# First linear attention of a fused attention chain: tile semaphores, another order of the products, other banks

## The chip, the cores and the metric

The kernel runs on one core of one Trainium2 chip. The metric is the device time of one execution in microseconds. The core has TensorE (PE), VectorE (DVE), ScalarE (ACT), GpSimd (POOL) and SyncE (SP), each with its own instruction queue in program order, and 16 DMA engines. The engines synchronise by semaphores.

## The reference

The computation is a chain over 8 batches of 576 positions. It has three stages; the first is the one that the change touches.

```python
kv  = einsum('bhsd,bhse->bhde', k, v)            # 8 heads of 64: one 64x64 state per head
out = einsum('bhsd,bhde->bhse', q, kv)           # linear attention
x   = out / sqrt(mean(out*out, -1) + 1e-6) * g_norm

# second stage: 4 experts, each a causal attention of head size 64 over x,
# of which the gate (x @ w_gate, two highest of four) mixes two
q, k, v = x @ wq[e], x @ wk[e], x @ wv[e]
ye = softmax(causal(q @ k.T / 8)) @ v @ wo[e]

# third stage
h = gelu(x @ w_in);  u, v = halves of h
v_s = w_sg @ layernorm(v) + b_sg                 # mixes positions
return x + (u * v_s) @ w_out
```

All inputs and the output are float32. In the third stage x stands for the output of the second.

## The kernel before, in words

The sequence of a batch is padded from 576 to 640 rows, five tiles of 128. The kernel is written with an order of work per batch ("part"), a list of units such as `("o", 3)`; every engine runs through the same list and does its own share of each unit, so the list sets the order on every queue. Part -1 is the opening (the list `FIRST`, line 79): it prepares the first batch and combines weights. Parts 0 to 7 are the batches; each ends with the first linear attention of the next batch.

PSUM is used in six slots: `w0` and `w1` of two banks each and `t0` to `t3` of one bank each. The class `Slots` (line 28) gives each unit a slot and counts two semaphores per slot: `full` is raised by PE when the unit's last matmul is done (`finish`), `free` by the engine that evicts last (`give`). PE waits in `dst` until the slot's former unit is evicted. In the opening the slots are written out in `FIRST_SLOT` (line 82); in the batches the four narrow slots go round. The first four units of batch 0 are the q/k products `("qk", (m, 0))`, in the slots t3, t0, t1, t2.

The units of the opening are:

- `woT`, `w2`: the output weights of the experts are transposed and multiplied with `w_in`, so that `wo @ w_in` is one weight. `("w2", c)` for c = 0 to 3 is one chunk of the contraction (eight matmuls of 512 columns, line 1050), accumulated in w0 and w1 over all four chunks.
- `kv`: the states of all heads for a batch, in slot t3 (line 1078). DVE copies them to `kvd`.
- `qT`, j: tile j of the queries is transposed by four PE transposes (line 1029) and evicted by ACT (line 569). The five tiles come by one DMA each (lines 381 and 384), and all raise the semaphore `q_loaded`; PE waits for all five before `("qT", 0)` (line 1026).
- `o`, j: queries times states (eight matmuls in the profile, line 1092). ACT squares it (line 593), DVE sums the squares per head (line 833), POOL raises to the power -1/2 (lines 513 and 514). ACT's square of tile j waits for DVE's sum of tile j - 1. DVE scales the tile (`scale_x`, line 731) and frees the slot; it does this one `o` unit late, behind the sum of the next tile (or at a later `x` unit), and for tile t of 2 or more it waits until `("x", t-2)` has been transposed, since there are two buffers.
- `x`, j: the scaled tile is transposed (line 1100), ACT evicts its rounded high half (line 597), DVE its low half (line 840), which frees the slot. All products of x are done in three passes over high and low halves.
- `split`, name: ACT writes the high half of a weight (line 575), DVE the low half (line 815). ACT waits for all DMAs of that weight; for the q/k weights (`wqk0` to `wqk3`) these are the eight DMAs of line 432.

A q/k product (line 1118, its matmuls at the helper's line 943) waits until the x tiles that it reads are evicted, its weight's halves are ready, and its slot is free. The values' products `v` wait for the weight `wv` in the same way.

SP issues the DMAs of the opening without waiting: `wo`, two chunks of `w_in`, k and v of batch 0, the five query tiles, two more chunks of `w_in`, g_norm, the q/k weights, the value weights. Then, once `kv` is done, follow `w_sg`, `w_out` and two small vectors, and, once `("qT", 4)` is done, sixteen DMAs of query blocks of batch 1 (line 392), which also raise `q_loaded`; DVE waits for them at `turn` in batch 0 (line 912).

Of the kernel before, what the change touches and what calls it, by code (L numbers as in the profile page):

```python
# [55 lines left out]
def moe_chain(nc, q, k, v, g_norm, w_gate, wq, wk, wv, wo, w_in, g_ln, w_sg, b_sg, w_out, out):  # L56
# [3 lines left out]
    PAD = P - S % P  # L60
    SP = S + PAD
    NT = SP // P
# [14 lines left out]


    FIRST = [("woT", 0), ("woT", 1), ("w2", 0), ("w2", 1)] + [("kv", c) for c in range(DC)]
    FIRST += [("qT", 0), ("qT", 1), ("o", 0), ("qT", 2), ("o", 1), ("qT", 3), ("qT", 4), ("o", 2), ("w2", 2), ("x", 0),  # L80
              ("split", "wqk0"), ("o", 3), ("x", 1), ("split", "wqk2"), ("w2", 3), ("o", 4), ("x", 2), ("x", 3), ("x", 4)]
    FIRST_SLOT = {("kv", 0): "t3", ("qT", 0): "t0", ("qT", 1): "t1", ("o", 0): "t2", ("qT", 2): "t0", ("o", 1): "t3",
                  ("qT", 3): "t1", ("qT", 4): "t0", ("o", 2): "t1", ("x", 0): "t0", ("o", 3): "t2", ("x", 1): "t3",
                  ("o", 4): "t1", ("x", 2): "t0", ("x", 3): "t2", ("x", 4): "t3"}


    LATE_QK = {0: [("split", "wqk1")], EP: [("split", "wqk3"), ("w2e", 0)], 1: [("split", "wv")]}
# [69 lines left out]
    def units(part):  # L157
# [3 lines left out]
        def ring(unit, among):  # L161
            if part < 0:
                got.append((unit, FIRST_SLOT[unit]))
                return
# [35 lines left out]
    with ExitStack() as ctx:  # L200
# [3 lines left out]
        def sem(name):  # L204
            return ctx.enter_context(nc.semaphore(name))
# [91 lines left out]
        wv_lo = sem("wv_lo")  # L297
        wo_lo = sem("wo_lo")
        wout_lo = sem("wout_lo")
        q_loaded = sem("q_loaded")  # L300
        q_turned = sem("q_turned")
        kv_loaded = sem("kv_loaded")
# [69 lines left out]
        def _(sp):  # L372
# [6 lines left out]

            def load_q(b):  # L380
                sp.dma_start(qin[PAD:P, 0, :].rearrange("p (h d) -> p h d", h=H),
                             q[b, :, 0:PAD, :].rearrange("h s d -> s h d")).then_inc(q_loaded, 16)
                for t in range(1, NT):
                    sp.dma_start(qin[:, t, :].rearrange("p (h d) -> p h d", h=H),
                                 q[b, :, P * t - PAD:P * (t + 1) - PAD, :].rearrange("h s d -> s h d")
                                 ).then_inc(q_loaded, 16)

            def load_q_blocks(b):

# [279 lines left out]
        def _(dve):  # L669
# [4 lines left out]
            def body(part):  # L674
# [4 lines left out]
                def src(unit):  # L679
                    u.wait_full(dve, part, unit)  # L680
                    return ps[u.slot(part, unit)]
# [110 lines left out]
                for kind, j in PLAN[part]:  # L792
                    U = (kind, j)
                    if U == ("kv", DC - 1):
                        U = ("kv", 0)
                        x = src(U)
# [9 lines left out]
                    elif kind == "woT":  # L806
                        x = src(U)
# [4 lines left out]
                    elif kind == "split":  # L812
                        dst, x, _, low_ready = split_w[j]
# [38 lines left out]
                    elif kind == "qk":  # L852
                        m, h = j
# [6 lines left out]
                    elif kind == "s":  # L860
                        if not 2 <= j < N - 2:
                            maximum(j, 0)
                            maximum(j, 1)
                    elif kind == "scale":
                        scale_probs(j, j + 1 if 2 <= j + 1 < N - 2 else None)
                    elif kind == "pv":
                        if j % 2 == 1:
                            t = j // 2
                            dve.wait_ge(yT_hi, count(part, NT, t + 1))
                            o = PAD if t == 0 and part % 2 else 0  # L870
                            give(nc.vector.tensor_tensor(  # L871
                                yT[:, LO, :, P * t + o:P * (t + 1)],
                                ps[u.slot(part, ("y", t))][:, 0:2 * P].rearrange("p (e n) -> p e n", e=EP)[:, :, o:P],
                                as_f32(yT[:, HI, :, P * t + o:P * (t + 1)]), ALU.subtract), ("y", t))
                    elif kind == "t2":
                        lo, hi = T_GROUPS[j // 2][1]
                        for a in range(2):
                            V = ("t", j, a, 1)
                            give(nc.vector.tensor_copy(pT[:, j % 2, a, P * lo:P * hi], src(V)[:, 0:P * (hi - lo)]), V)  # L879
                    elif kind == "gelu":  # L880
                        statistics(j)
                        if j >= 1:
                            normalise(j - 1)
                        if j >= 2:
                            vhat_low(j - 2)
                    elif U == ("u", 0):
                        normalise(NT - 1)
                        vhat_low(NT - 2)
                    elif U == ("u", 1):
                        vhat_low(NT - 1)  # L890
                    elif kind == "vs":
                        if part == 0 and j == 0:
                            dve.wait_ge(w_loaded["small"], 2 * 16)
                        if j >= 2:

                            dve.wait_ge(gT_lo, count(part, FC, j - 1))

                        give(nc.vector.scalar_tensor_tensor(  # L898
                            out=gt_tile[j % 2], in0=src(U)[:, W_LO:W_LO + S], scalar=gln_c[:, j:j + 1],
                            in1=bias_t[:, :], op0=ALU.mult, op1=ALU.add), U)  # L900
                        if j == FC - 1:

                            u.wait_drained(dve, part, ("u", j))
                            u.wait_drained(dve, part, U)
                            dve.wait_ge(gated_ready, count(part, FC, j))
                            nc.vector.tensor_tensor(gt_tile[j % 2], gt_tile[j % 2], qT_uT[:, j, PAD:SP],
                                                    ALU.mult).then_inc(gated_ready, 1)
                        if 1 <= j < FC - 1 or (j == FC - 1 and part == B - 1):
                            gated_low(j - 1)
                    elif kind == "turn":  # L910
                        if j == 0:
                            dve.wait_ge(q_loaded, 16 * NT + 256 * (part + 1))
                        dve.wait_ge(gated_ready, count(part, FC, j + 1))
                        nc.vector.transpose(qT_uT[:, j, PAD:SP], q_blocks[:, j, :]).then_inc(q_turned, 1)
                        if j == FC - 1:
                            gated_low(FC - 2)
# [9 lines left out]
        def _(pe):  # L926
            def body(part):
# [91 lines left out]
                for kind, j in PLAN[part]:  # L1019
                    U = (kind, j)  # L1020
                    if kind == "qT":

                        if j == 0:
                            if part < 0:
                                pe.wait_ge(q_padded, 1)
                            pe.wait_ge(q_loaded, 16 * NT)
                        x = dst(U)
                        for c in range(DC):
                            last = nc.tensor.transpose(x[:, P * c:P * (c + 1)], qin[:, j, P * c:P * (c + 1)], ident[:, :])
# [1 line left out]
                    elif kind == "woT":  # L1031
# [3 lines left out]
                        x = dst(U)  # L1035
# [5 lines left out]
                    elif kind == "w2":  # L1041
# [5 lines left out]
                        for c in range(EP):  # L1047
                            x = ps[u.slot(part, ("w2", c))]
# [5 lines left out]
                    elif kind == "wsgT":  # L1054
                        if j == 0:
                            pe.wait_ge(wsg_doubled, 1)
                        x = dst(U)
# [3 lines left out]
                    elif kind == "wsgR":  # L1061
                        x = dst(U)
# [4 lines left out]
                    elif kind == "kv":  # L1067
# [6 lines left out]
                        x = ps[u.slot(part, ("kv", 0))]  # L1074
# [8 lines left out]
                    elif kind == "o":  # L1083
# [6 lines left out]
                        x = dst(U)  # L1090
# [4 lines left out]
                    elif kind == "x":  # L1095

                        u.wait_drained(pe, part, ("o", j))
                        x = dst(U)
# [10 lines left out]
                    elif kind == "qk":  # L1109

                        m, h = j
                        o = PAD + HALF * h
# [81 lines left out]
```

## Time and profile before

| | us |
|---|---|
| median of 3 runs | 885.29 |
| lowest and highest | 882.73 and 887.86 |
| the profiled execution | 883.76 |
| its span, first to last instruction | 882.0 |
| PE busy | 849.6 (96%) |
| PE weight loads busy | 736.9 (84%) |
| DVE busy | 484.8 (55%) |
| ACT busy | 392.0 (44%) |
| POOL busy | 166.6 (19%) |

The busy time of PE counts its matmuls, which are pipelined and whose ends are modelled, so that it is no measure of how near PE is to its peak. The granted clock of PE has a mean of 0.996 over the span, where 1.00 is the level of 2.4 GHz and 0.50 that of 1.2 GHz. The span is 1.76 us shorter than the execution's time.

### The profile page before, as it was taken

Reading aid. Unit: us, or ns where it says so; the run is one execution under the profiler, and the core shown is the slowest. Engines: PE = TensorE matmul, PEld = TensorE weight load, DVE = VectorE, ACT = ScalarE, POOL = GpSimd, SP = SyncE. Lnnn points to the kernel's source line nnn. Section 1 sums busy time; section 2 is a strip of 40 time slices with the busy share of each in tenths; the row PEclk is TensorE's granted clock in tenths of the full one; section 3 lists DMA queues with packets and bytes.
Section 4 is the critical chain, followed back from the end, with each engine's and each line's share of the span. In section 5 each row is a group of like instructions: output and inputs, shape, how many; then the busy total and the mean of one; then the engine's idle time right before and its main releaser. Section 6 shows DMA issues by size and latency. Waiting matters only on the chain.

```text
span 882.0 us, 17155 instructions
## 1 busy us (share of the span) xinstructions
PE 849.6 (96%) x6797; PEld 736.9 (84%) x6797; DVE 484.8 (55%) x1257; ACT 392.0 (44%) x939; POOL 166.6 (19%) x205
## 2 busy tenths in 40 slices
PE   6798999999999999999999999999999999999898
PEld 3596798978989798987989789897998879897796
DVE  1558745476444755477443775447644575537740
ACT  0447533465234732465234652347423563246521
POOL 0402134002330033201330022400232002410220
PEclk9989999999999999999999999999999999999999
DMA  9910335003050032300331012500304000100001
GB/s 275 233 21 4 106 108 108 14 1 108 2 113 2 1 109 50 71 1 1 109 70 45 2 31 78 120 1 1 108 13 103 1 1 2 43 25 2 1 1 60
DMA packets 117407, 47.31 MB, mean 54 GB/s; under 512 B 94352, under 2 KB 110736, under 8 KB 117328
## 3 DMA queue, kind: packets, MB, share of 16 engines
q1 hardware_dynamic: 117328, 46.21, 21.0%
q8 instruction: 55, 0.90, 0.4%
q14 instruction: 24, 0.20, 0.1%
HBM read 35.19 MB, written 9.44 MB: 51 GB/s over the span
## 4 chain that ended last, share of the span: by engine, by line
PE 75%; DVE 12%; ACT 8%; SPq 2%; issue 1%; DMA 1%; POOL 0%; ACTq 0%; DVEq 0%
PE w L943 35%; PE t L943 20%; ACT probs L621 5%; PE t L997 4%; PE w L982 3%; PE t L1092 3%; DVE neg_max L739 3%; PE t L1013 3%; DVE probs L760 2%; PE t L1078 2%; PE w L1146 2%; PE t L1100 2%; ACT work L636 1%; DVE yT L871 1%; DVE big L788 1%
## 5 line engine op out<-in xcount | busy, mean ns | idle before, releaser
L943 PE MATMUL t<-big,wqk_s 128*128 128x288 f32 x768 | 112.4, 303 | 2.4 <-DVE big L840 1.7
L943 PE MATMUL w<-wout_s,big 128*128 128x512 f32 x432 | 108.1, 399 | 1.5 <-DVE big L788 0.5
L943 PEld LDWEIGHTS t<-big,wqk_s 128*128 128x128 f32 x768 | 105.4, 192 | 3.4 <-issue 2.3
L943 PE MATMUL w<-wsgT_s,big 128*128 128x288 f32 x768 | 107.7, 296 | 0.0
L943 PEld LDWEIGHTS w<-wsgT_s,big 128*128 128x128 f32 x768 | 104.3, 189 | 0.0
L621 ACT ACTIVATE probs<-w,neg_max 128x64 f32<-128x64 f32 (+4 forms) x160 | 83.0, 526 | 45.4 <-DVE neg_max L739 44.8
L943 PEld LDWEIGHTS w<-wout_s,big 128*128 128x128 f32 x432 | 79.6, 188 | 20.3 <-DVE big L788 3.2
L537 POOL TENSOR_TENSOR var_eps<-bn,eps_t 128x1 f32<-128x1 f32 x40 | 13.1, 328 | 413.3 <-DVE bn L776 412.6
L636 ACT ACTIVATE work<-t 128x384 f32<-128x384 f32 (+3 forms) x160 | 63.1, 450 | 44.8 <-PE t L997 42.7
L997 PE MATMUL t<-ident,probs 128*128 128x128 f32 x480 | 72.5, 282 | 7.1 <-DVE probs L760 6.0
L739 DVE TENSOR_REDUCE neg_max<-w 128x1 f32<-128x64 f32 (+4 forms) x160 | 74.0, 484 | 4.4 <-PE w L982 3.4
L997 PEld LDWEIGHTS t<-ident,probs 128*128 128x128 f32 x480 | 52.0, 140 | 26.5 <-DVE probs L760 15.9
L1013 PE MATMUL t<-work,vals 128*64 128x128 f32 x960 | 70.1, 281 | 2.1 <-DVE work L879 0.8
L655 ACT ACTIVATE big<-work 128x576 fp32r<-128x576 f32 x32 | 22.0, 687 | 111.9 <-POOL work L544 96.4
L898 DVE SCALAR_TENSOR_TENSOR work<-w,gln_c,bias_t 128x576 f32<-128x576 f32 x32 | 26.2, 818 | 79.5 <-PE w L943 78.6
L514 POOL TENSOR_TENSOR rms_inv<-ms,neg_half 128x8 f32<-128x8 f32 x40 | 65.7, 1641 | 3.1
L760 DVE TENSOR_SCALAR probs<-probs,row_inv,gate 128x64 f32<-128x64 f32 (+4 forms) x160 | 64.2, 444 | 2.9
L661 ACT ACTIVATE work<-w 128x512 f32<-128x512 f32 x36 | 21.5, 597 | 98.1 <-PE w L943 98.1
L1013 PEld LDWEIGHTS t<-work,vals 128*64 128x64 f32 x960 | 51.0, 136 | 16.4 <-issue 13.2
L982 PE MATMUL w<-big 64*128 64x288 f32 (+4 forms) x576 | 64.1, 328 | 0.0
L943 PE MATMUL t<-wv_s,big 128*128 128x260 f32 x480 | 61.7, 285 | 1.4 <-DVE yT L871 0.8
L833 DVE TENSOR_REDUCE ss<-squares 128x8 f32<-128x512 f32 x40 | 27.4, 684 | 61.9 <-ACT squares L593 61.9
(108 smaller groups left out, 1356.4 us busy)
## 6 DMA issues: line engine op xcount, KB each, us to landing
kin<-in_k_dram SPq DMA_DIRECT2D x8, 1024.0 KB, 6.2
vin<-in_v_dram SPq DMA_DIRECT2D x8, 1024.0 KB, 8.9
out_dram<-work SPq DMA_DIRECT2D x32, 256.0 KB, 2.1
qin<-in_q_dram SPq DMA_DIRECT2D x112, 72.0 KB, 2.4
staged_win<-in_moe_w_in_dram SPq DMA_DIRECT2D x4, 512.0 KB, 5.5
staged<-in_moe_w_sg_dram SPq DMA_DIRECT2D x4, 288.0 KB, 3.9
kin<-in_k_dram SPq DMA_DIRECT2D x8, 128.0 KB, 3.0
vin<-in_v_dram SPq DMA_DIRECT2D x8, 128.0 KB, 7.0
```

The costliest lines, as they stand in the source:

```text
L514: nc.gpsimd.tensor_tensor(rms_inv[:, j, :], ms[:, j, :], neg_half[:, 0:H], ALU.pow).then_inc(rms_ready, 1)
L621: exps = nc.scalar.activation(probs[:, j % 2, a, PAD:PAD + K], ps[slot][:, o:o + K], ACT.Exp, bias=neg_max[:, j, a:a + 1], accum_out=row_s ...
L636: give(nc.scalar.activation(pT[:, j % 2, a, P * lo:P * hi], x[:, 0:P * (hi - lo)], ACT.Copy), V)
L739: nc.vector.tensor_reduce(neg_max[:, n, a:a + 1], ps[slot][:, o:o + K], AX_X, ALU.max, negate=True).then_inc(max_ready, 1)
L760: last = nc.vector.tensor_scalar(x, x, row_inv[:, n, a:a + 1], gate[:, t, 2 * e + a:2 * e + a + 1], ALU.mult, ALU.mult)
L833: nc.vector.tensor_reduce(ss[:, j, :], sq_tile.rearrange("p (h d) -> p h d", h=H), AX_X, ALU.add).then_inc(ss_ready, 1)
L898: give(nc.vector.scalar_tensor_tensor(out=gt_tile[j % 2], in0=src(U)[:, W_LO:W_LO + S], scalar=gln_c[:, j:j + 1], in1=bias_t[:, :], op0=AL ...
L943: last = nc.tensor.matmul(o, stationary(hs, c), mv(hm, c), start=c == of[0] and p == 0, stop=c == of[-1] and p == len(PASSES) - 1)
L982: last = nc.tensor.matmul(ps[slot][:, o:o + w], big2[rows, hs, e, P * t:P * (t + 1)], big2[rows, hm, EP + e, PAD + k0:PAD + k0 + w], start ...
L997: last = nc.tensor.transpose(x[:, P * (b - lo):P * (b - lo + 1)], probs[:, n % 2, a, P * b:P * (b + 1)], ident[:, :])
L1013: last = nc.tensor.matmul(x[HD * a:HD * (a + 1), P * e:P * (e + 1)], vals[:, b, w:w + HD], pT[:, n % 2, a, P * b:P * (b + 1)], start=b == ...
L1092: last = nc.tensor.matmul(x[:, P * c:P * (c + 1)], qT_uT[:, c, P * j:P * (j + 1)], kvd[:, c, :], start=True, stop=True)
```

## The change

The list of the opening is reordered. The five `qT` and five `o` units follow each other with `qT` up to two units ahead, `("w2", 2)` moves from before `("x", 0)` and `("o", 3)` to between `("o", 3)` and `("x", 0)`, `("w2", 3)` moves from before `("o", 4)` to after `("x", 2)`, and `split wqk0` moves from after `("x", 0)` to before `("o", 3)`; `split wqk2` now stands after `("x", 2)`. The narrow slots of the opening are given out anew: `("x", 4)` leaves t3 for t0, and the last unit in t3 is now `("o", 4)`. Each query tile has a semaphore of its own (`q_first`), and PE waits before each `qT` for its own tile. `q_loaded` now counts only the query blocks. The batches' lists are not changed.

```diff
@@ -77,11 +77,11 @@
     FIRST = [("woT", 0), ("woT", 1), ("w2", 0), ("w2", 1)] + [("kv", c) for c in range(DC)]
-    FIRST += [("qT", 0), ("qT", 1), ("o", 0), ("qT", 2), ("o", 1), ("qT", 3), ("qT", 4), ("o", 2), ("w2", 2), ("x", 0),
-              ("split", "wqk0"), ("o", 3), ("x", 1), ("split", "wqk2"), ("w2", 3), ("o", 4), ("x", 2), ("x", 3), ("x", 4)]
-    FIRST_SLOT = {("kv", 0): "t3", ("qT", 0): "t0", ("qT", 1): "t1", ("o", 0): "t2", ("qT", 2): "t0", ("o", 1): "t3",
-                  ("qT", 3): "t1", ("qT", 4): "t0", ("o", 2): "t1", ("x", 0): "t0", ("o", 3): "t2", ("x", 1): "t3",
-                  ("o", 4): "t1", ("x", 2): "t0", ("x", 3): "t2", ("x", 4): "t3"}
+    FIRST += [("qT", 0), ("qT", 1), ("qT", 2), ("o", 0), ("qT", 3), ("o", 1), ("qT", 4), ("o", 2), ("split", "wqk0"),
+              ("o", 3), ("w2", 2), ("x", 0), ("o", 4), ("x", 1), ("x", 2), ("split", "wqk2"), ("w2", 3), ("x", 3), ("x", 4)]
+    FIRST_SLOT = {("kv", 0): "t3", ("qT", 0): "t0", ("qT", 1): "t1", ("qT", 2): "t2", ("o", 0): "t3", ("qT", 3): "t0",
+                  ("o", 1): "t1", ("qT", 4): "t2", ("o", 2): "t0", ("o", 3): "t2", ("x", 0): "t1", ("o", 4): "t3",
+                  ("x", 1): "t0", ("x", 2): "t1", ("x", 3): "t2", ("x", 4): "t0"}
     LATE_QK = {0: [("split", "wqk1")], EP: [("split", "wqk3"), ("w2e", 0)], 1: [("split", "wv")]}
@@ -297,6 +297,7 @@
         wv_lo = sem("wv_lo")
         wo_lo = sem("wo_lo")
         wout_lo = sem("wout_lo")
+        q_first = [sem(f"q_first_{t}") for t in range(NT)]
         q_loaded = sem("q_loaded")
         q_turned = sem("q_turned")
         kv_loaded = sem("kv_loaded")
@@ -379,11 +380,11 @@
             def load_q(b):
                 sp.dma_start(qin[PAD:P, 0, :].rearrange("p (h d) -> p h d", h=H),
-                             q[b, :, 0:PAD, :].rearrange("h s d -> s h d")).then_inc(q_loaded, 16)
+                             q[b, :, 0:PAD, :].rearrange("h s d -> s h d")).then_inc(q_first[0], 16)
                 for t in range(1, NT):
                     sp.dma_start(qin[:, t, :].rearrange("p (h d) -> p h d", h=H),
                                  q[b, :, P * t - PAD:P * (t + 1) - PAD, :].rearrange("h s d -> s h d")
-                                 ).then_inc(q_loaded, 16)
+                                 ).then_inc(q_first[t], 16)
             def load_q_blocks(b):
@@ -909,7 +910,7 @@
                             gated_low(j - 1)
                     elif kind == "turn":
                         if j == 0:
-                            dve.wait_ge(q_loaded, 16 * NT + 256 * (part + 1))
+                            dve.wait_ge(q_loaded, 256 * (part + 1))
                         dve.wait_ge(gated_ready, count(part, FC, j + 1))
                         nc.vector.transpose(qT_uT[:, j, PAD:SP], q_blocks[:, j, :]).then_inc(q_turned, 1)
                         if j == FC - 1:
@@ -1023,7 +1024,7 @@
                         if j == 0:
                             if part < 0:
                                 pe.wait_ge(q_padded, 1)
-                            pe.wait_ge(q_loaded, 16 * NT)
+                        pe.wait_ge(q_first[j], 16)
                         x = dst(U)
                         for c in range(DC):
                             last = nc.tensor.transpose(x[:, P * c:P * (c + 1)], qin[:, j, P * c:P * (c + 1)], ident[:, :])
```

## Rows read from the trace of the kernel before

**Rows 1.** The page, its second part: busy tenths in 40 slices, PE and its granted clock.

```profile
PE   6798999999999999999999999999999999999898
...
PEclk9989999999999999999999999999999999999999
```

**Rows 2.** The waits of PE from 80 us on: in total, times, the longest.

```profile
PE t L997 <- DVE probs L760: 5.7, 16, 0.5
```

**Rows 3.** The chain of waits in the first 100 us: start us, us, what.

```profile
10.86 2.76 SPq L384
...
15.49 5.13 DMA qin<-in_q_dram
...
27.10 3.44 PE w L1050 x8
...
33.74 0.61 DVE ss L833
...
36.43 0.69 DVE work L731
...
40.41 0.70 DVE work L731
```

**Rows 4.** The timeline of PE: start, us, engine, line, what, idle before and its releaser.

```profile
20.75 1.06 PE L1029 MATMUL t<-ident,qin 128*128 128x128 f32 x8 [1.68 <-DMA qin<-in_q_dram]
22.16 1.13 PE L1092 MATMUL t<-kvd,qT_uT 128*128 128x128 f32 x8 [0.34 <-ACT qT_uT L569]
23.13 0.60 PE L1029 MATMUL t<-ident,qin 128*128 128x128 f32 x4
...
37.27 0.63 PE L1100 MATMUL t<-ident,work 128*128 128x128 f32 x4 [0.20 <-DVE work L731]
41.16 0.66 PE L1100 MATMUL t<-ident,work 128*128 128x128 f32 x4 [3.26 <-DVE work L731]
43.47 7.51 PE L943 MATMUL t<-big,wqk_s 128*128 128x288 f32 x36 [1.66 <-DVE big L840]
51.20 1.82 PE L943 MATMUL t<-big,wqk_s 128*128 128x288 f32 x12 [0.22 <-issue]
...
54.16 6.02 PE L943 MATMUL t<-wv_s,big 128*128 128x260 f32 x48 [0.62 <-issue]
```

**Rows 5.** Three stretches: us, then busy us per engine, PEclk, DMA share, GB/s.

```profile
38.00:42.00 4.00, 0.66 (x4) 0.42 (x4) 2.33 (x4) 0.77 (x2) 3.07 (x6) 1.00 1.02 188
42.50:48.50 6.00, 5.03 (x21) 5.06 (x22) 1.89 (x3) 0.97 (x3) 0.00 (x0) 0.50 0.68 108
49.50:54.00 4.50, 3.82 (x32) 3.38 (x30) 3.83 (x6) 3.45 (x6) 0.00 (x0) 1.00 0.00 0
```

**Rows 6.** DMAs to landing (last number, us): third query tile; issue and landing of q/k weights.

```profile
qin<-in_q_dram SPq DMA_DIRECT2D x1, 256.0 KB, 7.4
...
25.54 0.51 SPq L432 DMA_DIRECT2D staged_wqk<-in_moe_wk_dram  x1
...
staged_wqk<-in_moe_wk_dram SPq DMA_DIRECT2D x1, 128.0 KB, 3.5
...
DMA to landing us min/median/max: 2.8/4.2/4.8
```

**Rows 7.** The timeline of ACT, then of DVE.

```profile
21.42 1.09 ACT L569 ACTIVATE qT_uT<-t 128x512 f32<-128x512 f32 x2 [19.40 <-PE t L1029]
23.33 0.60 ACT L593 ACTIVATE squares<-t 128x512 f32<-128x512 f32 x1 [0.82 <-PE t L1092]
...
24.74 0.60 ACT L593 ACTIVATE squares<-t 128x512 f32<-128x512 f32 x1 [0.33 <-DVE ss L833]
...
31.66 0.62 ACT L575 ACTIVATE wqk_s<-staged_wqk 128x512 fp32r<-128x512 f32 x1
...
49.44 0.41 ACT L605 ACTIVATE big<-t 128x288 fp32r<-128x288 f32 x1 [1.78 <-PE t L943]
...
31.79 0.75 DVE L840 SCALAR_TENSOR_TENSOR big<-t,gnorm_c,big 128x512 fp32r<-128x512 f32 x1 [2.50 <-ACT big L597]
```

## The prediction

> **What bounds the kernel now.** I read the page first [rows 1]: PE is busy for eight tenths or more of every slice but the first two, and its clock drops in one slice only, the third (44 to 66 us). From 80 us on PE's longest wait for anything is 5.7 us in total, for DVE's probabilities, and no DMA is among what it waits for [rows 2]. So the body of the kernel is PE work that the change does not touch, and whatever is won in the opening moves the rest ahead as a block. The opening is where to look.
>
> The chain of waits [rows 3] tells why the first q/k product begins only at 43.47. It starts with the queries' DMA, which lands at 15.49 + 5.13 = 20.62. Later it runs twice through DVE's reduction, POOL's power and DVE's scaling: the reduction that starts at 33.74 ends at 34.35, scaling starts at 36.43 (2.08 us for POOL's part); the next scaling starts at 40.41. Then come x4's transposes (41.16), its two evictions by ACT and DVE, and when DVE's is done the product, at 43.47 [rows 4]. PE has nothing to do meanwhile: it ends x3 at 37.90 and stands 3.26 us before x4. Two costs follow. The first is that idling. The second is its echo: the granted clock is 0.50 from 42.5 to 48.5, the 1.2 GHz level, and 1.00 from 49.5 [rows 5]. The first 36 matmuls of the q/k products take 7.51 us, the next 12 take 1.82 from first start to last end [rows 4], or about 1.65 in a row, so 36 would take about 5.0.
>
> **The change, part by part.** No instruction of the five engines is added or removed; SP issues the same DMAs in the same order. I rebuild the opening here on the new order from the durations of the old one.
>
> *One semaphore per query tile.* PE ends the state products (kv) at 19.08 and idles 1.68 us until the fifth tile lands [rows 4]. The third tile was issued at 10.86 [rows 3] and took 7.4 us to land (18.3) [rows 6], so three transposes can start at about 19.0; the other two have landed (20.62) before PE comes to them at 21.4 and 22.8. This alone moves the first state product from 22.16 to 20.4: qT0 at 19.0, its eviction 0.67 later (20.75 to 21.42) and 0.60 long, 0.14 to PE [rows 4, 7]. DVE's two copies of the state lie beside that eviction. But this doesn't count in the end, as will be seen.
>
> *State products ahead of the weight chunks.* From o0 at 20.4: 1.17 to the square (22.16 to 23.33); the next square follows 1.41 later (23.33 to 24.74), since it waits for DVE's reduction of this one: squares at 21.6, 23.0 and 24.4 [rows 4, 7]. PE needs 0.97 per o (22.16 to 23.13) and 0.46 per qT (eight matmuls in 1.06, four in 0.60) and has issued o3 by 25.2. The weight chunk w2/2 takes 3.44 [rows 3] to 28.6, x0 follows (its bank is free by then: POOL's powers of tiles 0 and 1 end about 2.0 after each reduction, 24.9 and 26.8, and scale 1 at 27.6), then o4 to 30.05. ACT, however, comes to split wqk0 at 25.0, in its order ahead of the square of tile 3, and that copy waits for all eight q/k weight DMAs. The last was issued at 25.54 and took 3.5 [rows 6]: 29.05. The old order had this copy at 31.66 [rows 7], where the wait cost nothing. Queued behind it are square 3, x0's eviction and all that DVE and POOL make of them. So the new chain is: landing 29.05; split starts 29.07, square 3 at 29.6 (a split is 0.62 long, and steps in a row overlap by 0.1, as the two evictions in 1.09 do) to 30.2; reduction 30.3; scale 2 30.9 to 31.6 (steps of 0.60 [rows 3]); x1 on PE 31.66, since it takes the bank that scale 2 frees; x0's low half (0.75 [rows 7]) ends at 32.3; x2 32.4 to 32.8; w2/3 to 36.2; x3, x4 to 37.1.
>
> The two POOL passes that were bare now lie beside this: tile 3's from the reduction's end at 31.0 to 33.0, tile 4's to 34.9, scale 4 to 35.6, all under w2/3. That is the cover; without it they would cost the 3.26 us of [rows 4] again. What PE still lacks is 1.6 us ahead of x1 and 0.3 ahead of x2.
>
> *The banks.* The first q/k product goes to t3, which x4 held and o4 holds now. It no longer waits for x4's two evictions (41.16 to 43.47, of which x4's transposes are 0.46: 1.85 us) but for scale 4, 35.6. So it starts at 37.1 where it was 43.47: 6.4 us. The second product needs t0, x4's bank, free at 39.0 (x4's 2.2 us of evictions after 36.7): it starts at 39.1, 0.35 late, and ends 1.85 later, at 40.95, if the clock stays at its higher level.
>
> *From there to the values.* In the old trace the eviction of that second product starts at 49.44 and the value product v0 at 54.16 [rows 4, 7], 4.72 later. This piece is a chain on ACT and DVE (weight halves, one after another), which the clock does not touch, so v0 goes to 40.97 + 4.72 = 45.7 from 54.16. The clock gives 2.1 us on top of the 6.4. Sum: **8.5 us**. From v0 on, order, banks and data are as before, the weight transfers are under way or landed by then (the query blocks, behind them in SP's order, are issued from 33.2), and the rest shifts.
>
> Against the profiled execution (883.76, span 882.0) this is 875.3; the median of the runs shown is 1.5 above that execution, 885.29, hence **876.8**.
>
> **Bounds.** The landing: the eight q/k weight transfers took 2.8 to 4.8 us [rows 6], so 28.3 to 30.3, one to one on the end: -0.7 to +1.3. Were the split hidden, x1 would be bound by x0 at 28.6 + 0.7 and scale 2, 30.1: 1.5 less; that is the floor. The clock: 0 to 3.4 us, half of the some 6.7 us for which it was low (more than 6 by [rows 5]). The other end of "the rest shifts" is that some of it is given back, below. Repeated runs differ by 2.5 us either way. A semaphore wait per tile in place of one I take at nothing: PE would otherwise be idle, and the next row's wait is 0.34; at most 5 x 0.14 = 0.7, ahead of a wait of 1.6. If the tile semaphores did nothing, o3 would end at 26.9, w2/2 at 30.4, x0's transposes at 30.9, and scale 2 could still go at 31.1: x1 0.2 later.
>
> **A rule of the skill against it.** The trace: ahead of the first qT and the first o PE idles 1.68 and 0.34 us [rows 4], and the clock stays at nine tenths or more in those slices [rows 1]; it is at 1.00 up to 42 and falls only after the 3.26 us without work and the pause behind x4 [rows 5]. The Trainium skill (TensorE: Matmul & The Clock Gate, "A second HAM failure mode: psum-queue depth-cycling") says that a kernel whose PE idles for short moments while it cycles through PSUM banks can have its clock swing between the two levels. Its rule would give rival A; by the trace I expect none.
>
> **Rivals.**
> A, the clock falls all the same (0.15). The new gaps (1.6 us before x1, then two short transposes) bring a low stretch like the old one, now over w2/3 and q/k products. For it: the fall came after x4's transposes, so behind work already resumed [rows 5]. Against: the old pause was twice as long. Gain 8.5 less 2.1 to 3.4: 5.1 to 6.4, 878.9 to 880.2 against the median.
> B, ACT waits longer at split wqk0 (0.09). The third query tile took 7.4 us; with such a latency the landing is 32.9 and 3.9 us of the gain go: 880.7. Against: the DMAs ahead of it are the same.
> C, the block does not shift whole (0.08): the sixteen query-block DMAs, issued 33.2 to 47, now lie beside more of the q/k products, whose evictions stretch. The waits after 80 us show no DMA, but the stretch to 80 may. Half the gain: 881 to 883.
> D, slower (0.06): the clock falls ahead of w2/3 and stays low while ACT and DVE prepare weights. Each us of it costs 0.5, so it must last 17 us (8.5 x 2) to eat all of the gain, and over 26 to make the kernel 0.5% slower: 890 and more. Against: PE was back at full clock by 49.5, after 6 us of unbroken products [rows 5].
>
> **How the numbers follow.** The forecast has 0.62. What a measurement can tell from no change is about 0.5%, 4.4 us. The forecast is outside it but for a tail, so is nearly all of A, and a third of B; C, most of B and those tails are within. Faster 0.76, same 0.18, slower 0.06. Range: from the floor and a low run, 872.8, over A up to the edge of B, 881.0.
>
> **What the profile will show.** qT0 directly behind kv at about 19.0, no wait for the query DMA; squares 0 to 2 1.4 us apart, then ACT idle from 25.0 to about 29.1 before split wqk0; x1 near 31.7; w2/3 between x2 and x3 with POOL's last two powers beside it; the first q/k product at about 37.1 with no DVE eviction before it; clock 1.00 throughout; v0 at about 45.7; the rest with unchanged sums. It would be wrong if ACT doesn't stand at the split (then more is won), if the clock shows a low stretch, or if q/k starts early and v0 doesn't.

## The result, and the profile after

| | us | runs |
|---|---|---|
| before | 884.85 (882.73 to 887.86) | 4 |
| changed | 874.62 (874.5 to 875.34) | 4 |
| ratio | 0.9891, 95% interval 0.9867 to 0.9914 | |

The forecast was 876.8 in 872.8 to 881.0: 8.5 us less. The change brought 10.2 between the medians and 9.3 between the two profiled spans, 882.0 and 872.7.

The waits of PE from 80 us on, in the changed kernel, answer to [rows 2]; the body is as it was.

```profile
PE t L998 <- DVE probs L761: 5.3, 15, 0.5
```

The timeline of PE, changed kernel (start, us, what, idle before). It answers to [rows 4]; its lines are one higher than before.

```profile
16.33 2.55 PE L1079 MATMUL t<-vin,kin 128*64 128x64 f32 x80
18.81 1.53 PE L1030 MATMUL t<-ident,qin 128*128 128x128 f32 x12
20.21 1.13 PE L1093 MATMUL t<-kvd,qT_uT 128*128 128x128 f32 x8
...
24.98 3.60 PE L1051 MATMUL w<-staged_win 128*128 128x512 f32 x8
28.42 0.60 PE L1101 MATMUL t<-ident,work 128*128 128x128 f32 x4
28.85 1.06 PE L1093 MATMUL t<-kvd,qT_uT 128*128 128x128 f32 x8
30.97 1.28 PE L1101 MATMUL t<-ident,work 128*128 128x128 f32 x8 [1.06 <-DVE work L732]
32.09 3.60 PE L1051 MATMUL w<-staged_win 128*128 128x512 f32 x8
35.53 1.04 PE L1101 MATMUL t<-ident,work 128*128 128x128 f32 x8
36.32 1.82 PE L944 MATMUL t<-big,wqk_s 128*128 128x288 f32 x12
38.44 3.40 PE L944 MATMUL t<-big,wqk_s 128*128 128x288 f32 x24 [0.30 <-DVE big L841]
...
45.01 6.02 PE L944 MATMUL t<-wv_s,big 128*128 128x260 f32 x48 [0.61 <-issue]
```

Three qT stand right behind kv, with no wait for a DMA. x1 follows after a pause of 1.06 us for scale 2, w2/3 lies between x2 and x3, and the first q/k product begins right behind x4. The 3.26 us ahead of x4 are gone. v0 begins at 45.01 in place of 54.16.

The chain of waits, changed kernel (start, us, what), in place of [rows 3]:

```profile
24.80 3.45 DMA staged_wqk<-in_moe_wk_dram
...
28.27 0.64 ACT wqk_s L576
...
28.93 0.52 DVE wqk_s L816
...
29.54 0.68 DVE ss L834
30.22 0.61 DVE work L732
...
30.97 0.63 PE t L1101 x4
```

No step of POOL is in it, nor the queries' DMA. It begins with the landing of the last q/k weight DMA at 28.25, goes over both halves of split wqk0 (ACT's high half, then DVE's low half), the sum of tile 3 and scale 2, and comes to x1. The low half stands ahead of the sum in DVE's order. The forecast had only square 3 there, which ends beside it (29.39, and the low half 29.45), so that nothing comes of it.

POOL's last two additions and powers (timeline of POOL, changed kernel) end at 34.10. They lie beside x1, x2 and the first 2 us of w2/3 (32.09 to 35.53):

```profile
30.30 0.20 POOL L514 TENSOR_TENSOR ms<-ss,eps_t 128x8 f32<-128x8 f32 x1 [1.81 <-DVE ss L834]
30.58 1.64 POOL L515 TENSOR_TENSOR rms_inv<-ms,neg_half 128x8 f32<-128x8 f32 x1
...
32.46 1.64 POOL L515 TENSOR_TENSOR rms_inv<-ms,neg_half 128x8 f32<-128x8 f32 x1
```

The granted clock (last number but two) of the changed kernel, from 30 to 46:

```profile
30.00:46.00 16.00, 13.88 (x88) 11.13 (x89) 12.34 (x21) 8.73 (x18) 4.92 (x8) 1.00 0.92 223
```

It does not leave the 2.4 GHz level, where [rows 5] had 0.50 for more than six microseconds.

### The profile page after: what moved, and what is told of

It is laid out like the page before. It is cut to its first block, busy times and chain, and to the rows that moved or that the text cites. A ratio compares the mean times of both kernels' runs of the same rounds, so it can differ in the third digit from the quotient of the medians.

```text
span 872.7 us, 17157 instructions
## 1 busy us (share of the span) xinstructions
PE 846.9 (97%) x6797; PEld 734.6 (84%) x6797; DVE 484.4 (56%) x1257; ACT 392.1 (45%) x939; POOL 166.6 (19%) x205
## 4 chain that ended last, share of the span: by engine, by line
PE 75%; DVE 12%; ACT 8%; SPq 3%; issue 1%; DMA 0%; ACTq 0%; DVEq 0%
PE w L944 35%; PE t L944 20%; ACT probs L622 5%; PE t L998 4%; PE w L983 3%; DVE neg_max L740 3%; PE t L1093 3%; PE t L1014 3%; DVE probs L761 2%; PE t L1079 2%; PE w L1147 2%; PE t L1101 2%; ACT work L637 1%; DVE yT L872 1%; DVE big L789 1%
## 5 line engine op out<-in xcount | busy, mean ns | idle before, releaser
L944 PE MATMUL t<-big,wqk_s 128*128 128x288 f32 x768 | 110.2, 298 | 1.1 <-DVE big L857 0.6
L944 PEld LDWEIGHTS t<-big,wqk_s 128*128 128x128 f32 x768 | 102.9, 188 | 2.0 <-issue 1.7
```

Of the source, the lines that this page charges most:

```text
L944: last = nc.tensor.matmul(o, stationary(hs, c), mv(hm, c), start=c == of[0] and p == 0, stop=c == of[-1] and p == len(PASSES) - 1)
```

## The experiments

Each profile is read at five places: the start of qT0, of x1 (in the old order, of x4), of the first q/k product and of v0, and the span. From v0 to the end all kernels take 827.7 to 828.0 us, so that v0 tells what a kernel gains. Medians and ratios come from several comparisons, and each ratio is to runs of the kernel before in the same one, so that medians of different comparisons (first and second run of the changed kernel, for instance) differ a little for that reason too.

The record also has the mean granted clock of every single run, and the runs of the kernel before differ in it. Of the 25 beside f1 to f4, twelve have a mean of 0.995 or 0.996 (median 882.87 us) and thirteen have 0.992 or 0.994 (886.75). With 0.50 as the low level, 0.996 over 881 us is by estimate 7 us of low clock, 0.994 is 11 and 0.992 is 14.

| kernel | qT0 | x1 or x4 | first product | v0 | span | median us | ratio to before |
|---|---|---|---|---|---|---|---|
| before | 20.75 | x4 41.16 | 43.47 | 54.16 | 882.0 | 884.85 | 1 |
| before again (g1) | 20.47 | x4 40.88 | 43.65 | 53.46 | 881.3 | 883.06 | 1.0 (0.9989 to 1.0011) |
| f1 tile semaphores alone | 19.66 | x4 40.10 | 42.87 | 52.76 | 880.6 | 881.82 | 0.9967 (0.995 to 0.9985) |
| f2 x4's bank alone | 20.32 | x4 40.73 | 41.49 | 51.85 | 879.7 | 881.0 | 0.9958 (0.9939 to 0.9976) |
| f3 pauses filled | 20.59 | x4 41.00 | 43.23 | 51.48 | 879.3 | 880.97 | 0.9964 (0.9946 to 0.9982) |
| changed | 18.81 | x1 30.97 | 36.32 | 45.01 | 872.7 | 874.62 | 0.9891 (0.9867 to 0.9914) |
| changed again (e1) | 19.89 | x1 31.18 | 36.53 | 45.23 | 873.0 | 875.34 | 0.9907 (0.9882 to 0.9932) |
| e2 one semaphore | 19.93 | x1 31.15 | 36.51 | 45.21 | 873.0 | 875.05 | 0.9896 (0.9879 to 0.9913) |
| e3 split late | 18.57 | x1 29.64 | 35.18 | 43.88 | 871.9 | 873.99 | 0.9885 (0.9866 to 0.9903) |
| e4 x4 in t3 | 19.01 | x1 31.07 | 38.55 | 48.25 | 876.2 | 877.93 | 0.9923 (0.9903 to 0.9943) |
| g2 the same, pause filled | 19.33 | x1 31.58 | 38.98 | 47.22 | 875.1 | 876.65 | 0.992 (0.9908 to 0.9932) |
| f4 all four splits early | 18.94 | x1 30.02 | 35.55 | 44.22 | 872.1 | 874.66 | 0.9888 (0.9853 to 0.9923) |
| g3 split late, x3/x4 banks | 19.87 | x1 30.95 | 36.48 | 44.70 | 872.5 | 874.08 | 0.9888 (0.9874 to 0.9903) |

### The changed kernel once more (e1)

No edit.

> The changed kernel once more, as the base for the three kernels that run with it. Theory (the opening is 9.2 us shorter and the rest shifts): 874.6 us, v0 (the value products) starts at 45.0 +- 0.7; what varies is the landing of the last q/k weight DMA, 28.3 to 29.1. Rival (the 0.65 us by which v0 came earlier than forecast belongs to the change, not to that landing): v0 stays at 45.0 whatever the landing.

v0 at 45.23. In this profile PE comes to qT0 1.08 us later than in the first one, and v0 is only 0.22 later. The split starts 0.22 later (28.49), and so does x1 (31.18). So the start of the opening is not in the chain and the landing is. In the first profile v0 came 0.7 us earlier than forecast (45.01 against 45.7) and the landing 0.80 earlier (28.25 against 29.05). That the one is the cause of the other follows from the chain; no run moved the landing alone. The transfer took what was forecast (3.45 against 3.5): it was the issue that came earlier, 24.80 against 25.54.

One of the five runs took 880.17. It is the only one with a mean granted clock of 0.996, the others have 1.00. So the clock falls in the changed kernel too, if seldom; that run was not profiled.

The end of w2/1 ahead of kv varies from run to run; the last section shows with what.

### One semaphore again (e2)

```diff
-                                 ).then_inc(q_first[t], 16)
+                                 ).then_inc(q_first[0], 16)
...
-                        pe.wait_ge(q_first[j], 16)
+                        if j == 0:
+                            pe.wait_ge(q_first[0], 16 * NT)
```

> Undoes one part: the five query tiles share one semaphore again and PE waits for all five before qT0; order and banks as changed. Theory (the tile semaphores are hidden behind ACT's wait for the q/k weights): qT0 moves from 18.8 to about 20.1, o3 and w2/2 end 1.3 us later, but the split starts at the same landing; x1 at most 0.4 us later, time +0.2 to +0.4 us. Rival (each us won at the first transposes counts): +1.3 us.

875.05 against 875.34, v0 45.21 against 45.23: nothing lost. In this profile kv happened to end as late as in e1, so PE did not wait for the tiles at all, and the profile alone proves little. That the median of six runs shows no loss either, and that e1 lost 1.08 us at qT0 and only 0.22 at v0, speaks against the 1.3 us of the rival. By these the semaphores are hidden in the new order. The forecast's bound of 0.2 us for them cannot be told from 0.

### split wqk0 late (e3)

```diff
-    ... ("qT", 4), ("o", 2), ("split", "wqk0"), ("o", 3), ("w2", 2), ("x", 0), ("o", 4), ("x", 1), ("x", 2), ("split", "wqk2"), ...
+    ... ("qT", 4), ("o", 2), ("o", 3), ("w2", 2), ("x", 0), ("o", 4), ("x", 1), ("x", 2), ("split", "wqk0"), ("split", "wqk2"), ...
```

> Moves one unit: split wqk0 from before o3 to after x2, so that ACT doesn't stand at it ahead of square 3. Theory (the chain from the weights' landing over square 3, its sum and scale 2 holds x1): ACT no longer idles from 24.8 to 28.3, x1 comes at 29.8 in place of 31.0, then everything 1.1 to 1.2 us earlier: time -1.1 us. Rival (x1 is bound by PE's own w2/2 and by DVE, and the wait at the split is beside it): 0 +- 0.2 us. Second rival (the two splits now in a row delay x3's eviction or the low halves): the gain is under 0.5 us.

x1 at 29.64 and v0 at 43.88, 1.13 earlier than in the changed kernel's first profile. The median is 1.35 less than e1's, which ran beside it (all five runs lie below all five of e1), and 0.63 less than that of the first four runs. The pause of PE ahead of x1 is gone (timeline of PE, late split):

```profile
28.61 1.06 PE L1093 MATMUL t<-kvd,qT_uT 128*128 128x128 f32 x8
29.64 0.63 PE L1101 MATMUL t<-ident,work 128*128 128x128 f32 x4
30.49 0.63 PE L1101 MATMUL t<-ident,work 128*128 128x128 f32 x4 [0.21 <-DVE big L841]
```

The split's wait did hold x1. What the late split hands on is the variation of the start: with it x1 comes 11.07, 11.08 and 11.08 us after qT0 (e3, f4, g3). With the split before o3, x1 comes 2.70, 2.69, 2.70, 2.69 and 2.69 after the split's start on ACT (changed, e1, e2, e4, g2), whenever qT0 was. The x1 of a run is the later of the two, so at x1 the late split would have won 0.2 in e1's run and 1.1 in the first. Some 0.2 of it is lost again behind x1: x2 waits 0.21 us for x0's low half, and v0 comes 14.24 us after x1 in place of 14.04. In the first run about 0.9 is left, in e1's nothing.

### x4 in t3 again (e4), and the same with PE's pause filled (g2)

```diff
-                  ("x", 1): "t0", ("x", 2): "t1", ("x", 3): "t2", ("x", 4): "t0"}
+                  ("x", 1): "t0", ("x", 2): "t1", ("x", 3): "t2", ("x", 4): "t3"}
```

> Undoes the part of the banks that counts: x4 goes into t3 again (behind o4), so that the first q/k product waits for both evictions of x4. Order and semaphores as changed. Theory: first q/k product at 38.3 in place of 36.3, but the second follows without its wait for t0 (38.4), so it ends at 41.6 in place of 40.1; v0 and the time +1.4 to +1.6 us, clock unchanged at 1.00. Rival (the values' products are bound by ACT's and DVE's weight halves whatever the banks): +0.3 us or less. Second rival (PE's pause of 2 us brings the clock down): +3 us or more.

In the second kernel of the pair PE has this in addition, ahead of the first product:

```diff
+                        if part == 0 and j == (0, 0):
+                            for r in range(14):
+                                nc.tensor.transpose(ps["t0"][:, P * (r % 4):P * (r % 4 + 1)], ident[:, :], ident[:, :])
```

> The changed kernel with x4 in t3 again, as in the experiment that cost 2.9 us, and 14 more transposes of the identity on PE in its pause of 1.9 us before the first q/k product (into t0, which the second product overwrites). Theory (of the 2.9 us, 1.4 to 1.6 are the later product and the rest is the clock): clock 1.00, first product at 38.4, v0 at 46.5, time +1.5 us against the changed kernel, 876.3. Rival (the later product alone costs all of it): +2.9 us, and the added transposes change nothing.

e4 took 877.93, 2.6 more than e1. From x1 to v0 it needs 17.18 us, the changed kernel 14.04 and g2 15.64. PE of e4, then two stretches of e4 (the clock is the last number but two):

```profile
35.64 1.04 PE L1101 MATMUL t<-ident,work 128*128 128x128 f32 x8
38.55 6.52 PE L944 MATMUL t<-big,wqk_s 128*128 128x288 f32 x36 [1.88 <-DVE big L841]
...
48.25 6.04 PE L944 MATMUL t<-wv_s,big 128*128 128x260 f32 x48 [0.62 <-issue]
```

```profile
39.00:42.00 3.00, 3.00 (x15) 3.00 (x14) 0.00 (x1) 0.52 (x2) 0.00 (x0) 0.50 0.74 108
43.00:46.00 3.00, 2.79 (x21) 2.58 (x20) 1.88 (x4) 2.47 (x5) 0.00 (x0) 1.00 0.84 135
```

And the same stretch of g2, with 14 more transposes (PE's timeline, then the stretch):

```profile
37.02 1.69 PE L1119 MATMUL t<-ident 128*128 128x128 f32 x14
38.98 3.42 PE L944 MATMUL t<-big,wqk_s 128*128 128x288 f32 x24 [0.26 <-DVE big L841]
```

```profile
39.00:42.00 3.00, 3.00 (x23) 3.00 (x24) 0.62 (x2) 0.93 (x2) 0.00 (x0) 1.00 0.88 118
```

One pause of 1.88 us brought the clock down: 15 matmuls in three microseconds against 23. With the pause filled by useless work the clock stays up and v0 follows x1 by 1.54 us less. So the bank of x4 is worth 1.6 us by itself (15.64 less 14.04) and another 1.5 by the clock. Of e4's six runs two took 876.34 and 876.58, with a mean granted clock of 1.00. The other four took 877.93 to 879.04, three of them with 0.997 or 0.998 and one (877.94) with 1.00. g2's six lie between 876.2 and 876.97, at 0.999 or 1.00. That fits a clock that falls in some executions and not in all, but for the run of 877.94, which nothing explains; only one of e4's was profiled.

### The semaphores alone, old order (f1)

```diff
+        q_first = [sem(f"q_first_{t}") for t in range(NT)]
...
-                                 ).then_inc(q_loaded, 16)
+                                 ).then_inc(q_first[t], 16)
...
-                            pe.wait_ge(q_loaded, 16 * NT)
+                        pe.wait_ge(q_first[j], 16)
```

> The kernel before with one part alone: a semaphore per query tile, old order and banks. Theory (in the old order nothing hides them, since split wqk0 comes at 31.7, well after the weights' landing): qT0 at 19.0, all of the opening 1.6 us earlier, x4 at 39.5 and v0 at 52.5; time -1.6 us. Rival (they are worth as little as in the new order): -0.4 us or less.

Ratio 0.9967, which is 2.9 us with 1.3 and 4.4 as ends; by profiles v0 is 0.7 and 1.4 earlier than in the two of before. In the old order x4 starts 20.41, 20.41, 20.41, 20.41 and 20.44 us after qT0 (before, g1, f2, f3, f1), so what qT0 gains reaches x4 in full. qT0 gained 0.8 to 1.1 here, since kv ended later than in the first profile. The theory holds; its size, 1.6, depends on how late kv is. The 2.9 us between the medians say more than that: all ten runs of f1 have a mean clock of 0.995 or 0.996, and before's twelve with the same clock have 882.87, which is 1.0 more. The rest belongs to before's runs with a lower mean clock. Why f1 had none of those in ten is open.

### The bank of x4 alone, old order (f2)

```diff
-                  ("o", 4): "t1", ("x", 2): "t0", ("x", 3): "t2", ("x", 4): "t3"}
+                  ("o", 4): "t1", ("x", 2): "t0", ("x", 3): "t2", ("x", 4): "t0"}
```

> The kernel before with one part alone: x4 in t0 in place of t3, so that the first q/k product does not wait for x4's evictions. Old order and semaphore. First product at 41.6 in place of 43.5 in either theory. If the clock is kept up by the shorter pause: second product at 43.5, v0 at about 50.0, time -4 us. If the clock falls at 42.3 all the same, since the 3.26 us pause before x4 is what brings it down: v0 at about 52.4, -1.7 us.

The first product follows x4 by 0.76 us in place of 2.31 and 2.77. The clock falls all the same, already at 39.5, in the 3.26 us pause:

```profile
39.50:46.00 6.50, 5.27 (x23) 5.28 (x24) 2.82 (x5) 1.62 (x3) 1.61 (x5) 0.50 0.85 135
```

From x4 to v0 it takes 11.12 us against 13.00 and 12.58: 1.5 to 1.9, the second of the two sizes named. The profiled run is one of five with a mean clock of 0.996 (881.51 to 882.49). The other five have 0.998, by estimate half as much low clock, and took 880.34 to 880.49, so that the shorter pause helps the clock in about half of the runs.

### PE's pauses filled, old order (f3)

```diff
+                        if part < 0 and j == 4:
+                            x = dst(U)
+                            for r in range(24):
+                                nc.tensor.transpose(x[:, P * (r % 4):P * (r % 4 + 1)], ident[:, :], ident[:, :])
                         u.wait_drained(pe, part, ("o", j))
...
+                        if part == 0 and j == (0, 0):
+                            for r in range(12):
+                                nc.tensor.transpose(ps["t0"][:, P * (r % 4):P * (r % 4 + 1)], ident[:, :], ident[:, :])
```

> The kernel before with 36 more transposes of the identity on PE and nothing else: 24 ahead of x4, in x4's bank, which x4 then overwrites, and 12 ahead of the first q/k product, in t0, which the second overwrites. They fill PE's two pauses (3.26 and 1.66 us) and make nothing earlier. Theory (the low clock is an echo of those pauses): clock 1.00 throughout, x4 at 41.2 and first q/k product at 43.5 as before, v0 at about 52.0 in place of 54.2, time -2.1 us although the kernel does more. Rival (the clock's fall has another cause, or it does not lengthen this stretch, since ACT and DVE bound it): 0 us, or up to +0.5 by the added work.

The kernel does 36 transposes more and its ratio is 0.9964: 3.2 us less, with ends 1.6 and 4.8. PE, old order with the pauses filled, and the clock from 42 to 48:

```profile
37.57 2.78 PE L1100 MATMUL t<-ident 128*128 128x128 f32 x24
41.00 0.66 PE L1104 MATMUL t<-ident,work 128*128 128x128 f32 x4 [0.64 <-DVE work L731]
41.49 1.47 PE L1122 MATMUL t<-ident 128*128 128x128 f32 x12
43.23 3.43 PE L943 MATMUL t<-big,wqk_s 128*128 128x288 f32 x24 [0.26 <-DVE big L840]
```

```profile
42.00:48.00 6.00, 5.53 (x41) 5.09 (x40) 2.69 (x5) 2.63 (x6) 0.00 (x0) 1.00 0.84 135
```

From x4 to v0 it takes 10.48 us in place of 13.00 and 12.58: 2.1 to 2.5 us are the clock's, and the pauses are its cause. The forecast's term was 2.1. The filling does not help in every run: eight of the ten have a mean clock of 0.999 or 1.00 (880.55 to 881.29), two have 0.998 (882.68 and 882.72). The median of the eight, 880.78, is 2.1 below that of before's twelve with 0.995 or 0.996.

### All four splits early (f4), and x3 and x4 in other banks (g3)

```diff
+              ... ("x", 2), ("split", "wqk0"), ("split", "wqk2"), ("split", "wqk1"), ("split", "wqk3"), ("w2", 3), ("x", 3), ("x", 4)]
...
+    LATE_QK = {EP: [("w2e", 0)], 1: [("split", "wv")]}
```

> The changed kernel with all four q/k weight splits after x2, before w2/3 (split wqk0 from before o3, wqk1 and wqk3 from batch 0). Theory: the 1.1 us of the late split, and 0.4 to 0.6 more, since the third and fourth product no longer wait for their halves and ACT reaches the value weights' half one split (0.5 us) earlier after the second product; time -1.6 us against the changed kernel, about 873.0 us, v0 at 43.4. Rival (DVE comes late to x3's low half and gives it back): no more than the late split alone.

In the other kernel, beside the late split:

```diff
-                  ("x", 1): "t0", ("x", 2): "t1", ("x", 3): "t2", ("x", 4): "t0"}
+                  ("x", 1): "t0", ("x", 2): "t1", ("x", 3): "t0", ("x", 4): "t2"}
```

> The changed kernel with split wqk0 after x2 and with x3 in t0 and x4 in t2, so that the second q/k product waits for x3's evictions in place of x4's. Theory (the value products hang on the second product's eviction, and that on its bank): no pause between first and second product, v0 0.3 to 0.45 us earlier than with the late split alone, at about 43.5; time 873.6 us, -1.5 against the changed kernel. Rival (PE or DVE give it back, as with the early halves): no more than the late split alone, 874.0.

Seen from x1, v0 comes after 14.24 us in e3, 14.20 in f4 and 13.75 in g3. The early halves win next to nothing. DVE makes four low halves in a row and comes late to x3's and x4's, and the second product waits for them. DVE, then PE, of f4:

```profile
34.09 2.48 DVE L816 TENSOR_TENSOR wqk_s<-staged_wqk,wqk_s 128x512 fp32r<-128x512 f32 x4
36.50 1.40 DVE L841 SCALAR_TENSOR_TENSOR big<-t,gnorm_c,big 128x512 fp32r<-128x512 f32 x2
```

```profile
38.04 4.97 PE L944 MATMUL t<-big,wqk_s 128*128 128x288 f32 x36 [0.67 <-DVE big L841]
```

The other banks win 0.49 us of this piece: there is no pause behind the first product. In the profiled run kv was 1.3 us late, the late split handed that on (x1 30.95), and v0 missed its forecast of 43.5 by it. The four runs took 872.65 to 874.34, those of e3 873.72 to 874.75: its shortest run is the shortest of all, but the two are not told apart by these. No version clearly beyond e3 came out.

### The kernel before once more (g1)

No edit.

> The kernel before once more, under a label of its own, for a second profile of it and for its spread (single runs so far 882.2 to 888.8, the changed kernel's 874.5 to 875.3 but for one). Theory A (the spread is the kernel's: the moment at which the clock falls and rises again differs from run to run): the runs spread over 2 to 6 us here too, the profile shows one low stretch of 5 to 8 us between 39 and 50, v0 at 53 to 55. Theory B (the spread belongs to the place of the comparison runs): the runs lie within 1.5 us at about 883.

Median 883.06, eight of the twelve runs at 882.45 to 883.18 and four at 885.15 to 885.56. The low clock lies at 40.5 to 47.0 here, 2 us earlier than in [rows 5]:

```profile
40.50:47.00 6.50, 4.46 (x18) 4.10 (x19) 1.73 (x3) 0.78 (x2) 0.76 (x3) 0.50 0.89 152
```

More of it falls on the pauses, and v0 is 0.7 earlier, of which 0.28 is the earlier qT0. Theory A holds in part: the spread belongs to the kernel, but is about 3 us. The mean granted clocks tell where it comes from: the eight shorter runs have 0.995 or 0.996, the four longer ones 0.992 or 0.994. That is by estimate 11 to 14 us of low clock in place of 7. Where in the kernel it lies is open, since none of the longer runs was profiled.

## Why the prediction was right

**Where the time is.** Right. The opening up to v0 is 9.15 us shorter by the profiles, the span 9.3. The rest shifted whole: 827.84 us from v0 to the end before, 827.69 after. Rival C has nothing for it: from x1 to v0 it took 14.04 us, which is the forecast's own figure (45.7 less 31.66), and from v0 on nothing grew.

**The semaphores.** Right in both halves. PE reaches qT0 earlier by them (18.81 for 19.0 forecast), and they count only where nothing else is later: e2's kernel without them loses nothing, f1's gains by them. What I didn't foresee is that kv's own end moves by 1.3 us between runs (qT0 at 18.57 to 19.89 in the new order), and that this decides what they win.

**The wait at split wqk0.** Right, and measured: the split starts at the landing, x1 comes 2.70 after it where 2.6 was forecast (31.66 less 29.07). x1 came at 30.97 because the landing was 28.25, inside the bound of 28.3 to 30.3 but for 0.05; the same size of shift is seen in v0. That bound took the time of issue as fixed and let the transfer vary, and it was the other way round: the last weight DMA was issued at 24.73 to 27.47 in the thirteen profiles and took 3.4 to 3.8 us. In the profiles of the new order it had landed by 28.25 to 29.0; in g1, with the same DMAs in the same order, at 30.9. By estimate such a landing would have cost the changed kernel 2.6 us (30.9 less 28.25), so that the early one was also luck. The floor of 1.5 us for a hidden split was too high: e3's v0 is 1.13 earlier, 0.24 of which is its earlier qT0, and 0.2 goes to x2's wait for x0's low half.

**The state products ahead of the chunks.** Right: POOL's last two powers lie beside x1, x2 and w2/3, the first product begins 5.35 us after x1 in place of the forecast 5.4. No run takes back the order alone. The nearest is e4, which keeps the new order with x4 in its old bank: its v0 (48.25) comes 5.9 and 5.2 us before those of the two profiles of before. As e2 finds nothing for the semaphores, that is the order's part, together with a low clock of 3.4 in place of 6.8 us; it is a difference, not a test.

**The banks.** The direct part is right: 1.85 forecast, 1.6 in the new order (g2), 1.5 to 1.9 in the old (f2). The second product waited 0.30, 0.35 forecast. From the second product's eviction on ACT to v0 it took 4.71 us (40.30 to 45.01) where 4.72 was forecast, so the carried-over piece holds.

**The clock.** The term was right, 2.1 forecast, 2.1 to 2.5 by f3, and 2.0 by the pieces from the first product to v0 (10.69 and 8.69). The cause, PE's pauses, is shown by filling them. What was wrong is the argument on rival A, that the clock falls only after the 3.26 us and the pause behind x4, and once work has resumed. In g1, f1 and f2 it falls inside the pause of 3.26 us, before x4, and f2 has no pause behind x4. e4 has one pause of 1.88 and the clock falls. The changed kernel's longest pause near this place is 1.06, so the margin is thinner than I said: had x4 stayed in t3, 1.5 us would have gone by the clock beside the 1.6 of the later product. And one of the changed kernel's nine runs, the 880.17 of e1, does have the lower mean clock. Rival A, at 0.15, did come about in one run of nine. The Trainium skill (TensorE: Matmul & The Clock Gate, "What's actually happening") says that the clock is throttled by default, that activity releases it, and that the moment of the change varies from run to run; the traces agree. In the two profiles of before the clock falls at 42.2 and 40.5, and every profile's opening starts with PE at half its later rate, for a time that varies (last section).

**Against the median.** The forecast of 8.5 against 10.2 measured, or 876.8 against 874.62: some 0.7 us is the landing, and the rest the choice of the anchor. I added to both kernels the 1.5 us by which before's median lay above its profiled execution (883.76), but the changed kernel's median lies only 0.12 above its own (874.5). Before's medians in four comparisons are 883.5 to 884.9. Its longer runs have a lower mean clock (g1), and the changed kernel's stay within a microsecond but for the one of 880.17. So it is likely that about a microsecond of the gain between the medians is low clock that before has in a part of its runs and the changed kernel nearly never; by profiles, which are of runs with 0.996 and 1.00, the gain is 9.3.

## What to carry to other kernels

Find for each edit what would be late if it worked: in the new order PE reached the first transposes up to 1.9 us earlier and nothing of it came out at the end, since a weight copy in ACT's queue waited for a DMA that lands later; moving that one copy won about 0.9 more. Give a bank that the next stage needs first to the unit whose eviction ends first, and price it with the clock: a later first product, with a pause of 1.9 us on PE, cost 1.6 us by itself and another 1.5 by the clock. Two profiles of one kernel tell what a chain hangs on: when its start moves and its end doesn't, the start is not in it. And look at the mean clock of each run before reading a difference of medians: f1's 2.9 us are 1.0 between runs of like clock.

## What the runs showed of the hardware that I had not expected

- The granted clock fell to 0.50 for some 3.4 us behind a single pause of PE of 1.88 us (e4, from 38.9). Up to the pause PE had been busy for 5.5 of 6.5 us (30.0 to 36.5). Around the pause of 3.26 us it was low for some 6.8 us (before, g1, f1, f2).
- PE reached qT0 between 18.57 and 19.89 us in kernels whose instructions are the same up to there; the sixteen matmuls of the first two weight chunks took from 8.86 us (e3) to 10.14 (e1), without a wait that the profile names. In all thirteen profiles these matmuls begin at half rate: their weight loads take 0.34 us and stand 0.85 apart, and from some moment on they take 0.19 and stand 0.43 apart. The moment is 10.84 in e3 and 13.44 in e1, three more long steps, which is the whole difference. The granted clock reads 1.00 throughout this stretch. That PE is at its lower clock here all the same is argued from the factor of two, and not shown. Timeline of weight loads, e3, then e1:

```profile
9.99 0.34 PEld L1051 LDWEIGHTS w<-staged_win 128*128 128x128 f32 x1 [0.52 <-issue]
10.84 0.19 PEld L1051 LDWEIGHTS w<-staged_win 128*128 128x128 f32 x1 [0.51 <-issue]
```

```profile
12.59 0.34 PEld L1051 LDWEIGHTS w<-staged_win 128*128 128x128 f32 x1 [0.52 <-issue]
13.44 0.20 PEld L1051 LDWEIGHTS w<-staged_win 128*128 128x128 f32 x1 [0.52 <-issue]
```

- The last q/k weight DMA landed between 28.25 (changed) and 30.9 us (g1), although SP issues the same DMAs in the same order and without waiting. What varied was the time of its issue, 24.73 (e2) to 27.47 (g1).
